# Slot inputs of a soft mixture of experts, weighted batch by batch with a running maximum inside the next batch's MLP

## The reference, cut to what matters

```python
attn_out = _attn_ref(q, k, v, f)                  # 4 batches, 8 heads, 576 tokens, 64 wide
x = transpose(attn_out).reshape(2304, 512)
h = x @ w_in;  x = (h * sigmoid(1.702 * h)) @ w_out       # 512 -> 2048 -> 512

logits = x @ phi                                  # 2304 tokens x 32 slots
d = exp(logits - logits.max(0));  d /= d.sum(0) + 1e-09   # over all 2304 tokens
slot_input = d.T @ x                              # 32 x 512
for e in range(8):                                # 4 slots each, 512 -> 1024 -> 512
    slot_out[e] = maximum(slot_input[e] @ w1[e], 0) @ w2[e]
c = exp(logits - logits.max(1));  c /= c.sum(1) + 1e-09   # over the 32 slots
return c @ slot_out                               # 2304 x 512
```

## Time and profile before

| | |
|---|---|
| median of 3 runs | 763.99 us (762.84 to 764.31) |
| the profiled execution, its time | 763.06 us |
| the profiled execution, its span | 761.3 us |
| PE busy | 711.8 us, 94% of the span |
| DVE, ACT, POOL busy | 58%, 57%, 52% |
| start of the last x2t eviction | 686.91 us |
| first expert matmul | 701.91 us |
| last expert's down | 739.89 us |
| last result row copied | 752.76 us |

### The profile page before, as it was taken

The page is one execution under the profiler, slowest core; times in us unless marked ns, Lnnn a source line. Parts: engine busy times, 40 slices in busy tenths (PEclk is TensorE's granted clock), DMA queues, the critical chain, the costliest instruction groups (busy, mean ns, idle before and its releaser), DMA issues.

```text
span 761.3 us, 15776 instructions
## 1 busy us (share of the span) xinstructions
PE 711.8 (94%) x6027; PEld 677.7 (89%) x6027; DVE 444.2 (58%) x1255; ACT 436.6 (57%) x1031; POOL 399.2 (52%) x439
## 2 busy tenths in 40 slices
PE   3899979999999999999999999999999999998983
PEld 3888879999999998999999989999999999995652
DVE  5898857676677656675666557766542332225413
ACT  4788866575757675666666675857563344331113
POOL 3355357474747755565757554757375576530000
PEclk9999989999999999999999999999999999999997
DMA  4433323332333333233421413332113545399986
GB/s 104 107 92 107 93 67 91 86 94 82 96 95 95 95 85 91 80 111 78 113 77 48 131 45 95 95 95 80 56 56 106 167 133 198 131 362 375 396 321 248
DMA packets 96506, 96.65 MB, mean 127 GB/s; under 512 B 61296, under 2 KB 61296, under 8 KB 96432
## 3 DMA queue, kind: packets, MB, share of 16 engines
q1 hardware_dynamic: 96432, 95.66, 41.0%
HBM read 90.84 MB, written 4.79 MB: 126 GB/s over the span
## 4 chain that ended last, share of the span: by engine, by line
PE 77%; DVE 9%; ACT 7%; DMA 3%; issue 2%; POOL 0%; SPq 0%; DVEq 0%; POOLq 0%
PE mb L1204 52%; PE yb L1057 6%; PE zb L1076 5%; PE xb L1103 5%; DMA ring_b<-in_moe_w 2%; PE xb L1037 2%; ACT prob L689 2%; DVE ptl L844 1%; DVE prob L838 1%; ACT xh L713 1%; PE mb L1256 1%; PE yb L1059 1%; DVE kl L806 1%; DVE qs L802 1%; PE yb L1295 1%
## 5 line engine op out<-in xcount | busy, mean ns | idle before, releaser
L1204 PE MATMUL mb<-xh,wih 128*128 128x288 f32 x512 | 159.0, 310 | 7.8 <-DVE xl L855 4.3
L1204 PE MATMUL mb<-gh,woh 128*128 128x288 f32 x512 | 156.5, 306 | 3.2 <-DVE x2t L932 3.2
L1204 PE MATMUL mb<-xl,wih 128*128 128x288 f32 x512 | 151.5, 296 | 0.0
L1204 PE MATMUL mb<-xh,wil 128*128 128x288 f32 x512 | 151.4, 296 | 0.0
L1204 PE MATMUL mb<-gl,woh 128*128 128x288 f32 x512 | 150.8, 294 | 0.0
L1204 PE MATMUL mb<-gh,wol 128*128 128x288 f32 x512 | 150.8, 294 | 0.0
L643 POOL TENSOR_TENSOR gl<-hid,gh 128x288 fp32r<-128x288 f32 x128 | 105.2, 827 | 74.6 <-ACT gh L730 72.9
L925 DVE SCALAR_TENSOR_TENSOR hid<-gate,mb 128x288 f32<-128x288 f32 x128 | 57.7, 451 | 116.2 <-ACT gate L736 115.1
L660 POOL TENSOR_TENSOR wol<-stage,woh 128x512 fp32r<-128x512 f32 x64 | 82.6, 1291 | 62.2 <-ACT woh L675 62.2
L689 ACT ACTIVATE prob<-prob,m_row 64x576 f32<-64x576 f32 (+4 forms) x160 | 96.5, 604 | 32.8 <-DVE m_row L824 31.9
L660 POOL TENSOR_TENSOR wil<-stage,wih 128x512 fp32r<-128x512 f32 x64 | 82.1, 1290 | 56.6 <-ACT wih L675 56.5
(11 more groups left out here) (196 smaller groups left out, 1462.0 us busy)
## 6 DMA issues: line engine op xcount, KB each, us to landing
stage<-in_moe_w_in SPq DMA_DIRECT2D x64, 256.0 KB, 3.0
stage<-in_moe_w_out SPq DMA_DIRECT2D x64, 256.0 KB, 2.6
ring_a<-in_moe_w SPq DMA_DIRECT2D x16, 1024.0 KB, 7.9
ring_b<-in_moe_w SPq DMA_DIRECT2D x14, 1024.0 KB, 13.0
cum_b<-cum_dram SPq DMA_DIRECT2D x32, 288.0 KB, 3.6
qk_in<-in_q SPq DMA_DIRECT2D x32, 144.0 KB, 3.0
qk_in<-in_k SPq DMA_DIRECT2D x32, 144.0 KB, 3.4
v_in<-in_v SPq DMA_DIRECT2D x32, 128.0 KB, 3.2
```

The source lines that it names most:

```text
L1204: ins = mm(bank[:, 0:HALF], a[:, t, P * (j % 4):P * (j % 4) + P], x[:, t, cols], start=(i == 0), stop=(i == 11))
```

## The change

The slots' weighting is done batch by batch. It needs no maximum over all tokens: `low_max[:, m+1]` holds the negated maximum per slot over the batches up to m, and all earlier sums are scaled by `kept` = exp(old maximum - new maximum). The maxima are held per partition (column group by slot), so each of the four groups has a maximum of its own until the end.

- For batches 0 to 2, in the next MLP: DVE takes the maximum of the transposed logits `lt` behind unit 2 (`slot_max`). ACT takes the exponentials `et`, with their sum, and `kept` at unit 3. PE turns `et` back to tokens by slots behind unit 7 ("turn_e"), and ACT copies them to `ewt`. Behind unit 9, "send" multiplies the batch's five token tiles by them (five fp32 matmuls of 512 columns, groups 0 to 3 and again 0); DVE adds the result to the scaled `acc`.
- `x2tok` holds one batch (5 tiles instead of 15), and `x2last`, `logits`, `gm` and `ew` are gone. This gives two more ring places: `ring_x` is free from the start and takes matrix 0 in batch 1's MLP, and there are five `ring_a`. So matrices 0 to 5 are loaded by the end of the last MLP (ten half loads there instead of eight), 6 to 10 at its end, and 11 to 15 reuse places.
- The last batch: "post" 0 behind unit 61 (logits and transposes of tiles 0 and 1), "post" 1 behind unit 62 (of the transposes of tiles 2 to 4, the two feature blocks that are ready), "post" 2 behind unit 63 (the rest). The logits of tiles 0 and 1 wait for two DVE memsets of their bank. DVE's maximum and ACT's exponentials read the logits from PSUM.
- Behind it: `top_row`, `row` and `top_back` take the maximum over the four groups and spread it again; `factor` scales each group; the denominator is one matmul with `blk4`; factor and reciprocal go into `sel_f`, by which the four slot matmuls scale. The last batch's combine weights are worked out later, behind the first expert's first copies.
- The memsets of `mb` and `yb` ahead of the experts are gone, and POOL clears `acc` at the start instead of `x2tok`.

```diff
+TURN_E_AT = 7
+SEND_AT = 9
+MAX_AT = 2
+EXP_AT = 3
+FIRST_EXPERT_AT = (18, 34)
-SOFTMAX_AT = (8, 9, 10, 11, 18, 19, 20, 21)
+SOFTMAX_AT = (10, 11, 18, 19, 20, 21)
-BUSY = (9, 3, 14)
+BUSY = (2, 3, 3)
...
-    return (held_steps(m) + mlp_steps(m, 0, U_MLP - 2) + [(0, ("post", 0))]
-            + mlp_steps(m, U_MLP - 2, U_MLP) + [(0, ("post", 1))])
+    return (held_steps(m) + mlp_steps(m, 0, U_MLP - 2) + [(0, ("post", 0))] + mlp_steps(m, U_MLP - 2, U_MLP - 1)
+            + [(0, ("post", 1))] + mlp_steps(m, U_MLP - 1, U_MLP) + [(0, ("post", 2))])
...
-                    if last and j == 2:
+                    if isinstance(m, int) and m == 1 and u in FIRST_EXPERT_AT:
+                        load_half_expert(0, FIRST_EXPERT_AT.index(u))
+                    if last and u % 6 == 2 and u // 6 < 2 * len(ring_a):
...
+            def exponentials(m, x):
+                act.wait_ge(max_made, m + 2)
+                wait_from(act, e_turned, m)
+                nc.scalar.activation(et[:, :], x[:, 0:P + 64], ACT.Exp, bias=low_max[:, m + 1:m + 2],
+                                     accum_out=bsum[:, m:m + 1]).then_inc(e_made, 1)
+                nc.scalar.activation(kept[:, m:m + 1], low_max[:, m:m + 1], ACT.Exp, scale=-1.0,
+                                     bias=low_max[:, m + 1:m + 2]).then_inc(kept_made, 1)
...
+            act.wait_ge(top_spread, 1)
+            act.wait_ge(top_made, 1)
+            nc.scalar.activation(factor[:, :], top_back[:, 0:1], ACT.Exp, bias=top[:, 0:1]).then_inc(factor_made, 1)
+            nc.scalar.copy(x2tok[:, 3, P * AHEAD:MODEL], last_tokens[3][:, P * AHEAD:MODEL]).then_inc(token_out, 1)
...
+                elif st == ("post", 0):
+
+                    dve.wait_ge(acc_made, 1 + m)
+                    dve.wait_ge(lt_made, 1 + m)
+                    nc.vector.memset(last_logits[32:64, P:P + 64], -3e38)
+                    nc.vector.memset(last_logits[64:P, P:P + 64], -3e38).then_inc(lt_made, 1)
...
+            def keep_sent(m, bank):
+                dve.wait_ge(kept_made, m + 1)
+                dve.wait_ge(acc_made, 1 + m)
+                nc.vector.scalar_tensor_tensor(out=acc[:, :], in0=acc[:, :], scalar=kept[:, m:m + 1], in1=bank,
+                                               op0=ALU.mult, op1=ALU.add).then_inc(acc_made, 1)
...
+            def send(bank):
+                for i in range(QT):
+                    g, r = i % 4, QW[i]
+                    ins = mm(bank[32 * g:32 * g + SLOTS, :], ewt[0:r, i, :], x2tok[0:r, i, :],
+                             start=(i < 4), stop=(i in (1, 2, 3, 4)), skip_group_check=True)
+                return ins
```

More of the change, by code:

```diff
@@ L109, in mlp_steps @@
             steps.append((-1, ("turn", 0)))
+        elif m and u == TURN_E_AT:
+            steps.append((-1, ("turn_e", 0)))
+        elif m and u == SEND_AT:
+            steps.append((-1, ("send", 0)))
     return steps
@@ L144, in bank_order @@
                 order.append(("turn", m - 1, 0))
+            elif m and u == TURN_E_AT:
+                order.append(("turn_e", m - 1, 0))
+            elif m and u == SEND_AT:
+                order.append(("send", m - 1, 0))
     return order
@@ L337, in build @@
         so4 = sb("so4", [P, MODEL], F32R, tail_b)
+        hx = sb("hx", [P, 2, 256], F32, tail_b)
+        hxt = sb("hxt", [P, 2, 2, P], F32, tail_b)
+        so_t = sb("so_t", [P, KM, 4, SLOTS], F32, tail_b)
+        top = sb("top", [P, 1], F32, tail_b)
+        row = sb("row", [1, 4, SLOTS], F32, tail_b)
+        row_s = sb("row_s", [1, SLOTS], F32, tail_b)
+        factor = sb("factor", [P, 1], F32, tail_b)
+        part_sum = sb("part_sum", [P, 1], F32, tail_b)
+        den = sb("den", [P, 1], F32, tail_b)
+        rden = sb("rden", [P, 1], F32, tail_b)
+        sel_f = sb("sel_f", [P, SLOTS], F32, tail_b)
         tail_b.close()
         NOUT = BATCH * QT
-        room = x2last[:, :, :].rearrange("p i n -> p (i n)")
-        hx = room[:, 0:512].rearrange("p (e n) -> p e n", e=2)
-        hxt = room[:, 512:1024].rearrange("p (e c n) -> p e c n", e=2, c=2)
-        so_t = room[:, 1024:1536].rearrange("p (t r s) -> p t r s", t=KM, r=4)
-        ring = ring_a + ring_b + [ring_x[:, :]]
+        ring = [ring_x[:, :]] + ring_a + ring_b
         NR = len(ring)
@@ L461, in bank_of @@
             if m == BATCH - 2 and kind != "unit":
-                return last_tokens[i] if kind == "token" else yb[:, 0, :] if kind == "logits" else zb[:, 0, :]
+                if kind == "token":
+                    return last_tokens[i]
+                return {"logits": yb[:, 0, :], "turn": zb[:, 0, :], "turn_e": zb[:, 1, :], "send": xb[:, 0, :]}[kind]
             return mb[:, place[kind, m, i] % 2, :]
@@ L790, in _ @@
             nc.vector.tensor_scalar(f_sb, f_sb, 1e-4, 1.0, ALU.max, ALU.min).then_inc(f_clip, 1)
-            nc.vector.memset(ones[:, :], 1.0)
             nc.vector.memset(carrier[:, :], 0.0).then_inc(unit_out, 2)
@@ new lines, in _ @@
+            dve.wait_ge(den_added, 1)
+            nc.vector.reciprocal(rden[:, :], den[:, :]).then_inc(den_added, 1)
+            dve.wait_ge(den_added, 2)
+            nc.vector.tensor_scalar(sel_f[:, :], sel4[:, :], factor[:, 0:1], rden[:, 0:1], ALU.mult, ALU.mult
+                                    ).then_inc(sel_scaled, 1)
+            dve.wait_ge(sent, m + 1)
+            keep_sent(m, last_sent)
+            dve.wait_ge(slots_summed, 1)
+            nc.vector.tensor_copy(slot_t[:, :, :], slot_ps[:, 0:KM * SLOTS].rearrange("p (t s) -> p t s", t=KM)).then_inc(slot_made, 1)
@@ L1167, in wait_bank @@
                     pe.wait_ge(o_sum, BATCH * HEADS)
+                    if kind in ("turn", "turn_e", "send"):
+                        pe.wait_ge(token_out, QT * m + QT)
                     return
@@ new lines, in _ @@
+            pe.wait_ge(row_made, 2)
+            mm(top_back[:, 0:1], row[:, :, :].rearrange("o g s -> o (g s)"), ident[0:1, 0:1], start=True, stop=True
+               ).then_inc(top_spread, 1)
+            busy(BUSY[1], last_sent)
+            pe.wait_ge(ewt_made, m + 1)
+            pe.wait_ge(token_out, QT * (m + 1))
+            send(last_sent).then_inc(sent, 1)
+            pe.wait_ge(sel_made, 1)
+            pe.wait_ge(den_in, 1)
+            mm(top_row[:, 0:1], blk4[:, :, :].rearrange("p g s -> p (g s)"), part_sum[:, :], start=True, stop=True
+               ).then_inc(den_made, 1)
```

358 lines of the change are left out of this document (213 added, 145 removed).

## The result

| | before | after |
|---|---|---|
| median of the runs | 764.12 us (762.84 to 764.31) | 773.84 us (771.97 to 774.5) |
| ratio of the medians, 95% interval | | 1.0127 (1.0106 to 1.0148) |
| span of the profiled execution | 761.3 us | 770.1 us |
| start of the last x2t eviction | 686.91 us | 702.22 us |
| first expert matmul | 701.91 us | 711.34 us |

The account below looks back on a forecast made before the run. PE time inside the MLPs and the chain behind the last unit bound it, weight arrival only for experts 5 to 7. +6.5 + 0.8 + 0.8 - 6.1 - 2.1 = -0.1 on 763.99 gave 763.9 us, range 760.2 to 766.8.

Parts of the forecast that it names:

- Part 1: Work moved into three MLPs: turn_e and send 2.06 each time, 0.3 for ACT waits, unit shift 0; +6.5 us.
- Part 2: End of the last MLP: logits wait for two DVE memsets, +0.8; six transposes now before unit 63, +0.8 us.
- Part 3: Chain behind the last unit to the first expert matmul: 8.9 us in place of 15.0, a gain of 6.1.
- Part 4: Expert weights: more matrices loaded early, so PE never waits at experts 5 to 7; -2.1 us.
- (a): Slower, in ACT's queue: exponentials and ewt copies delay token copies and tanh, 1.2 per attention MLP; 766.3 us, chance 0.18.
- (b): Faster, in the send: the fifth tile overlaps, so a send costs 0.9, four times; 760.3 us, chance 0.13.
- (c): At the experts: the weights still end last, so the 2.1 are not gained; 766.0 us, chance 0.07.
- (d): In three MLPs' sends: array runs empty at each tiling switch, 0.2 us twice a send; 765.1 us, chance 0.10.

Follow-up runs that it names:

- the marks of the experiment: Changed kernel with DVE's two memsets of the logit bank moved from behind unit 61 to behind unit 50 of the last MLP: 772.0 us, ratio 1.01.
- the spread send: Changed kernel with the send's fifth tile cut into four 128-column pieces, one per column group (sums not the same): 772.79 us, ratio 1.011.

## Why the prediction was wrong, by its own steps

**The step that failed** is the last sentence of Part 1: the other MLP units shift by one place against the attention steps, "I take 0 for that, plus or minus 0.5". It costs 1.62 in each of two MLPs, 3.2 in all (2.4 between the medians), and the experiment with two empty steps shows that nothing else is needed for it. The prediction looked at what queues behind the new steps in the MLP's first ten units, and took the units behind them as unchanged. The order of the two kernels showed unit 20 going from ahead of the qk transposes to behind them. The question to put there was whether DVE, with two steps to do ahead of `xst`, needed the 1.6 us that the unit had given it.

**Terms mis-sized.** The send takes 1.97, not 1.8: the scale was the dispatch's 0.90 a round over twenty matmuls, and a lone round takes 0.98 or 0.99. turn_e takes 0.40 and makes the unit behind it 0.11 longer, not 0.26 in all: the scale was eight transposes in a row, and two have the start of the row to pay. Together 2.54 by the marks (2.48 by these rows) in place of 2.06, three times: 1.4. Nothing of it lay beside other work, as the prediction said. The 0.3 that it added for waits behind ACT did not come.

**Missed altogether.** The eight selector copies (four had stood in the tail at 693.5, with 0.17 each, and four are new) appear nowhere in the prediction, neither as a DVE cost nor as a wait: 1.5 to 1.6. Their own 1.5 us would have been hidden, as behind unit 46. The GpSimd splits beside them made the cost, and these could have been looked up in GpSimd's timeline for that quarter.

**Part 2** had the mechanism and the size: 0.97 for the memsets (0.8 forecast, 0.9 to 1.1 by the marks of the experiment), and the last MLP's remaining 3.34 agrees with 2.54 for send and turn_e and 0.8 for the six transposes.

**Part 3** was right, 5.88 for 6.1, with the send held by ACT's copy of tile 3 as said.

**Part 4** had the mechanism right and the size wrong: 1.30 for 2.1. Of its three places only one gave its gain, the wait of 1.20. One (0.41 in expert 5's down) shows no sign of a wait for weights, since it stays at 2.32 with them in place, and one (0.28) has a second wait of 0.26 just under it.

**The rivals.** (a) said slower, which came, but not by its mechanism: PE's waits at the turn are the same before and after (0.78 at 288.61 and 288.88), so ACT's queue costs nothing new. (b) fell: the fifth tile does not overlap. (c) fell. (d) was not borne out, though its 0.4 an MLP is near the 0.48 that send and turn_e cost over the forecast: two more drains a send would have shown as idle or as a send of 2.2; it is 1.97, and the spread send is 1.35 and without a gap. Whether part of the 0.17 over 1.8, or of the 0.11 behind turn_e, comes from a switch stays open. The Trainium skill, "TensorEngine Tiling (Array Packing)", section Key Properties, has the rule of a drain at a change of the mode; no run here shows a price for it. None of the rivals was the shift, though the prediction named it as an uncertainty and gave it half a us.

**What adds up.** Shift 3.2, sends and turn_e 1.4, less the 0.3 for ACT that did not come; selector copies 1.5 to 1.6, experts 0.8, memsets 0.2 to 0.3, the stretch behind the last unit 0.2: 7.1 to 7.3 of the 8.9 us between forecast and span. Of the rest, 0.27 at the start and 0.57 in batch 1's MLP differ from one execution to the next in kernels of the same order, so they are scatter of the one execution profiled. The 0.67 behind the last down is not scatter: from there to the end it takes 20.98 to 21.41 in the four kernels with the old tail and 21.7 to 22.4 in the twelve with the new one, whose stores are issued over 0.7 us more. The forecast had 0 for it, and why the stores are slower stays open. Some 0.2 is left. The median lies another 1.9 above the profiled execution, which was the fastest of the four, where it lay 1.1 above it before; half clock at the first expert in part of the executions would do that, but no run shows it for this kernel.

## What to carry to other kernels

Where a list of steps is spread over another by weights, a step of small weight moves every later step of the list: print both orders to the end, and at each place where a unit leaves the front of a wait, ask how long the engine waited for needed that unit's time. Work moved off a chain into a stage where TensorE is 98% busy pays its whole length there, three times here for one time saved. For DVE copies from SBUF to SBUF, look at what GpSimd does beside them before you place them.

## What the hardware showed that was not expected

- A DVE copy of 32 x 128 or 32 x 32 elements takes 0.17 to 0.22, and 1.37 or 1.19 when GpSimd has begun a 128 x 512 elementwise step (1.28) just ahead of it. The trace shows the wait as part of the copy's own duration, not as idle time.
- TensorE's granted clock fell to 0.50 (1.2 GHz) at the first expert in the profiled executions of eight kernels, with either tail, and stayed at 1.00 in eight others. The 32 matmuls then took 2.59 to 3.60 in place of 1.91. PE had been busy for some nine tenths of the 2 us ahead in one kernel where it fell, and for six tenths in one where it did not; what decides it stays open. The old tail has waits for weights behind it, which one would expect to hide part of it, and they hid next to nothing: from the first expert to the last down it took 38.64 and 39.17 with first experts of 2.59 and 3.19, against 37.98 and 38.14 with 1.91.
- The same fall in the result stage, which fillers do prevent, costs nothing that the medians show; the stores behind it take 12 to 13 us either way.
